# A causal convolution and two gated layers on one core: the convolution's steps spread over both phases of a tile, and eight input buffers allocated at another place

## The chip, the cores and the metric

One core of a Trainium2 chip runs the whole kernel. The metric is the device time of one execution in microseconds (us); less is better. The four compute engines run side by side and are ordered only by semaphores: TensorE (PE, with its weight loads shown apart as PEld), VectorE (DVE), ScalarE (ACT) and GpSimd (POOL). SyncE (SP) issues all DMAs.

## The reference, cut to what matters

```python
# x: 4 x 4096 x 192, weight: 8 x 7 (8 heads of 24 channels, 7 taps)
w = softmax(weight, axis=-1)
x[t, channel] = sum over k of w[head, k] * x[t - 6 + k, channel]   # zero before the sequence
x = x.reshape(16384, 192)
h = x @ w_in1;  x = (h * cos(h)) @ w_out1               # 192 -> 2048 -> 192
h = x @ w_in2;  out = (h * clip(h + 3, 0, 6) / 6) @ w_out2
```

All in float32.

## The kernel before, in words

The 16,384 tokens are cut in 32 tiles of 512. Everything on the chip is transposed: channels (or hidden units) on partitions, 512 tokens along the row. 192 channels are 128 ("main") and 64 ("tail").

**Precision.** Each float32 operand of a product is held as a rounded high part and a low part (the remainder), and a product is made of high x high, low x high and high x low. So `in_f` (float32) gives `in_hi` and `in_lo`, and `in_ftail` gives `in_tail` and `in_twin`; the gated hidden values in `gate` give `g_hi` (by ACT) and `g_lo` (by POOL).

**Phases and slots.** A phase is one layer of one tile, cut in 8 slots (`SLOTS`); a slot makes 2 x 128 of the 2048 hidden units. The order of phases is L1 tile 0, L1 tile 1, L2 tile 0, L1 tile 2, L2 tile 1, and so on: a "turn" k is L1 of tile k followed by L2 of tile k-1 (`turn_phases`). In a slot PE makes the first products (`first_unit`, L374, out to `h_ps`) of this slot and the second products (`main_unit` L381 to `acc`, `tail_unit` L388 to `acc_tail`) of the slot three before (`LAG`). All matmuls use 64 rows of the array, and two of them run at once, one on the lower 64 partitions and one on the upper 64. `phase` on PE walks 19 rounds (`TURNS`) per slot, each round one `lower` and one `upper` matmul; in 18 of the 19, one of the two is a first product and the other a second product. In all there are 512 slots of 19 rounds, 9728 rounds.

**From h to g.** For L1: ACT copies h with a bias to an integer (L523), DVE subtracts (L628), ACT takes the cosine (L533), DVE multiplies (L639). For L2: ACT adds 3 and clips below (L525), DVE clips above and multiplies (L642). Then ACT rounds to `g_hi` (L540) and POOL subtracts to `g_lo` (L794).

**What PE waits for.** Before the first products of a slot PE waits for `g_ready`: DVE must have gated the first half of the slot two before, since `h_ps` has two places. At slot 0 of a phase it also waits for `lo_ready` and `twin_ready`: the phase's inputs must have been split. For L1 of the next tile these are `in_hi`, `in_twin`, `in_tail` (ACT, `split_high`, L552, L555, L558) and `in_lo`, the lower half of `in_tail` (DVE, `split_low_main` L695 and `split_low_tail` L700).

**The convolution.** For each tile DVE transposes the loaded x (`turn_x`, L657 and L658), puts in the 6 columns kept from the tile before (`put_halo`, L672 and L673), and does 14 steps (`conv_taps`): 7 taps, each on main and on tail. Steps 0 and 1 are a product (L683), the other 12 a product and a sum, scalar_tensor_tensor (L687). All of this is placed by hand: in DVE's L2 phase, `turn_x` and `put_halo` behind slot 0's gating, then 3 steps in each of slots 1 to 4 and 2 in slot 5 (`conv_from=1`, `rate=3`). The splits stand at slot 6 (`SPLIT_SLOT = SLOTS - 2`) on ACT and DVE. In slot 3 (`DRAIN_SLOT`) DVE also drains the accumulators of the phase before (`drain_acc`), in slot 7 (`TURN_SLOT`) it transposes a finished output tile (`turn_result`). In the first phase (L1 tile 0) there are 2 steps a slot, with 4 done ahead.

**SP's queue.** In the loop, turn k issues the load of x for tile k+1 and then the store of tile k-2. A load of tile i waits for `x_turned`: x of tile i-1 must have been transposed. A store waits for `o_turned`.

**At the start** the weights are loaded and split, and PE does 10 dummy matmuls (`warm_up`, L499, 128 rows each) between the 9th step of the first convolution and the first product.

**Buffers.** On a partition they lie one behind the other in the order of their allocation, each rounded up to 32 bytes. The weights, `g_hi` and `g_lo` all begin at byte 128 of a 512-byte line. Between them and the split inputs stand `xT` and `xT_tail` (2072 bytes each) and `halo` and `halo_tail` (888 bytes each), so that `in_hi`, `in_lo`, `in_tail` and `in_twin` begin at byte 448. Every slice of weights that PE loads begins a multiple of 512 bytes into its buffer.

Of the kernel before, what the change touches and what calls it, by code (L numbers as in the profile page):

```python
# [14 lines left out]
P = 128  # L15
TOK = 512
LAG = 3
WARM_PRODUCTS = 10
WARM_STEP = 9
# [10 lines left out]
Phase = namedtuple("Phase", "layer tile base before number result convolved conv_from rate setup source")  # L30


def conv_moe_kernel(nc, x, weight, w_in1, w_out1, w_in2, w_out2, out):
# [60 lines left out]
    with ctx:  # L94
# [21 lines left out]
        stage = sb("stage", [P, 2, W])  # L116

# [10 lines left out]
        in_hi = [sb(f"in_hi{n}", [P, TOK], F32R) for n in (1, 2)]  # L128
        in_lo = [sb(f"in_lo{n}", [P, TOK], F32R) for n in (1, 2)]
        in_tail = [sb(f"in_tail{n}", [P, TOK], F32R) for n in (1, 2)]  # L130
        in_twin = [sb(f"in_twin{n}", [P, TOK], F32R) for n in (1, 2)]
# [120 lines left out]
        SPLIT_SLOT = SLOTS - 2  # L252
        TURN_SLOT = SLOTS - 1
        TURNS = 19
        STEPS_AHEAD = 4
# [32 lines left out]

        def first_phase():
            return Phase(L1, 0, 0, None, 0, None, 1, 1, 2, 0, L2)  # L290

        def turn_phases(k):

            base = 2 * SLOTS * k - SLOTS
            first = isinstance(k, int) and k == 1
            last = isinstance(k, int) and k == TILES - 1
            return [Phase(L1, k, base, L1 if first else L2, 2 * k - 1, None, None, None, None,
                          1 if first else None, L1),
                    Phase(L2, k - 1, base + SLOTS, L1, 2 * k, None if first else k - 2,
                          None if last else k + 1, 1, 3, 2 if first else None, L2)]  # L300

        def last_phase():
            return Phase(L2, TILES - 1, END - SLOTS, L2, 2 * TILES - 1, TILES - 2, None, None, None, None, L1)
# [7 lines left out]
        @block.sync  # L311
        def _(sp):
            def load_x(i):

                if not isinstance(i, int) or i > 0:
                    sp.wait_ge(x_turned, 2 * i)
                for b in range(BLOCKS_D):
                    sp.dma_start(chip_block(x_in, x_in_tail, b), dram_block(x_blocks, i, b)).then_inc(x_loaded, 16)

            def load_block(b):  # L320
                for dst, src in loads_of(b):
                    sp.dma_start(dst, src).then_inc(staged[buffer_of(b)], 16)
# [12 lines left out]
            load_x(1)  # L335
            for b in (6, 7):
                sp.wait_ge(wlo_done, b - 5)
                load_block(b)
            for b in (8, 9):
                sp.wait_ge(wlo_done, b - 1)  # L340
                load_block(b)
            load_x(2)
            for b in range(10, 2 * BLOCKS):
                sp.wait_ge(wlo_done, b - 1)
                load_block(b)
            with sp.Fori(2, TILES - 1) as k:
                load_x(k + 1)
                store(k - 2)
            for i in range(TILES - 3, TILES):
                store(i)  # L350
            sp.wait_ge(o_stored, 16 * (BLOCKS_D * TILES + 1))

        @block.tensor
        def _(pe):
# [138 lines left out]

            def warm_up():

                pe.wait_ge(whi_done, 1)
                pe.wait_ge(conv_step, WARM_STEP)
                for _ in range(WARM_PRODUCTS):
                    pe.matmul(h_ps[:, 1, TOK:W], win_hi[L1][:, 0:P], win_hi[L1][:, 0:TOK], start=True, stop=True)  # L499
# [7 lines left out]
            with pe.Fori(2, TILES - 1) as k:  # L507
                for ph in turn_phases(k):
                    phase(ph)
            for ph in turn_phases(TILES - 1):  # L510
                phase(ph)
# [4 lines left out]
        def _(act):  # L516
# [54 lines left out]
            def phase(ph):  # L571
                for q in range(SLOTS):
# [6 lines left out]
                    if ph.convolved is not None and q == SPLIT_SLOT:  # L579
# [33 lines left out]
            with act.Fori(2, TILES - 1) as k:  # L613
                for ph in turn_phases(k):
                    phase(ph)
            for ph in turn_phases(TILES - 1):
                phase(ph)
# [4 lines left out]
        def _(dve):  # L622
# [80 lines left out]
            def phase(ph):  # L703
                for q in range(SLOTS):
# [67 lines left out]
            for n in range(STEPS_AHEAD):  # L772
# [4 lines left out]
            with dve.Fori(2, TILES - 1) as k:  # L777
                for ph in turn_phases(k):
                    phase(ph)
            for ph in turn_phases(TILES - 1):  # L780
                phase(ph)
# [69 lines left out]
```

## Time and profile before

| | us |
|---|---|
| three runs | 2375.68, 2374.58, 2376.42 (median 2375.68) |
| the profiled execution | 2375.52 |
| its span (first to last instruction) | 2373.8 |
| mean granted TensorE clock | 0.997 of full |

| engine | busy us | share of the span | instructions |
|---|---|---|---|
| PE | 2286.3 | 96% | 19470 |
| PEld | 1997.7 | 84% | 19470 |
| DVE | 1851.5 | 78% | 2509 |
| ACT | 1705.8 | 72% | 2836 |
| POOL | 1468.8 | 62% | 1059 |

A matmul's busy time is a modelled 0.39 us, while in a full stream one starts every 0.23 us, so PE shows as busy through short waits; the starts tell more than the shares. A turn of the loop takes 72.36 us.

### The profile page before, as it was taken

Reading aid. Unit: us, or ns where it says so; the run is one execution under the profiler, and the core shown is the slowest. Engines: PE = TensorE matmul, PEld = TensorE weight load, DVE = VectorE, ACT = ScalarE, POOL = GpSimd, SP = SyncE. Lnnn points to the kernel's source line nnn. Section 1 sums busy time; section 2 is a strip of 40 time slices with the busy share of each in tenths; the row PEclk is TensorE's granted clock in tenths of the full one; section 3 lists DMA queues with packets and bytes.
Section 4 is the critical chain, followed back from the end, with each engine's and each line's share of the span. In section 5 each row is a group of like instructions: output and inputs, shape, how many; then the busy total and the mean of one; then the engine's idle time right before and its main releaser. Section 6 shows DMA issues by size and latency. Waiting matters only on the chain.

```text
span 2373.8 us, 57021 instructions
## 1 busy us (share of the span) xinstructions
PE 2286.3 (96%) x19470; PEld 1997.7 (84%) x19470; DVE 1851.5 (78%) x2509; ACT 1705.8 (72%) x2836; POOL 1468.8 (62%) x1059
## 2 busy tenths in 40 slices
PE   5899999999999999999999999999999999999998
PEld 4789798888889888888898888998788988888886
DVE  8688877888877888777888778887778887788853
ACT  5876777766777667777667777677776677776674
POOL 6766666566566666566666665665666666656664
PEclk9999999999999999999999999999999999999999
DMA  4100000000000000000000000000000000000001
GB/s 109 37 8 15 0 13 13 13 13 7 7 13 13 13 13 0 13 13 13 13 9 4 13 13 13 13 0 13 13 13 13 12 1 13 13 13 13 2 7 21
DMA packets 208238, 32.94 MB, mean 14 GB/s; under 512 B 203088, under 2 KB 207184, under 8 KB 208208
## 3 DMA queue, kind: packets, MB, share of 16 engines
q1 hardware_dynamic: 208208, 32.53, 7.8%
q8 instruction: 20, 0.33, 0.1%
q14 instruction: 10, 0.08, 0.0%
HBM read 19.92 MB, written 12.58 MB: 14 GB/s over the span
## 4 chain that ended last, share of the span: by engine, by line
PE 44%; issue 22%; DVE 19%; POOL 9%; ACT 4%; DVEq 1%; POOLq 0%; SPq 0%; DMA 0%; ACTq 0%
PE h_ps L374 18%; PE acc L381 16%; PE acc_tail L388 11%; POOL g_lo L794 9%; DVE in_ftail L687 6%; DVE gate L642 5%; DVE in_f L687 4%; DVE in_f L683 1%; DVE in_tail L700 1%; ACT in_tail L558 1%; DVE in_ftail L651 1%; ACT in_hi L552 1%; ACT in_twin L555 1%; ACT pre L525 1%; ACT g_hi L540 0%
## 5 line engine op out<-in xcount | busy, mean ns | idle before, releaser
L794 POOL TENSOR_TENSOR g_lo<-gate,g_hi 128x512 fp32r<-128x512 f32 x1024 | 1428.9, 1417 | 857.1 <-ACT g_hi L540 855.7
L381 PE MATMUL acc<-g_hi,wout 64*128 64x512 f32 x4096 | 1429.9, 389 | 1.7 <-POOL g_lo L794 1.7
L374 PE MATMUL h_ps<-in_hi,win_hi 64*128 64x512 f32 x2048 | 808.3, 395 | 60.8 <-DVE in_tail L700 46.5
L540 ACT ACTIVATE g_hi<-gate 128x512 fp32r<-128x512 f32 x1024 | 613.7, 631 | 326.4 <-DVE gate L642 275.6
L381 PEld LDWEIGHTS acc<-g_hi,wout 64*128 64x128 f32 x4096 | 756.2, 185 | 66.4 <-issue 3.1
L388 PE MATMUL acc_tail<-g_lo,wout 64*128 64x512 f32 x2048 | 807.4, 394 | 0.0
L388 PE MATMUL acc_tail<-g_hi,wout 64*128 64x512 f32 x2048 | 805.6, 393 | 0.0
L374 PE MATMUL h_ps<-in_lo,win_hi 64*128 64x512 f32 x2048 | 803.2, 392 | 0.0
L374 PE MATMUL h_ps<-in_hi,win_lo 64*128 64x512 f32 x2048 | 800.3, 391 | 0.0
L381 PE MATMUL acc<-g_lo,wout 64*128 64x512 f32 x2048 | 800.2, 391 | 0.0
L374 PE MATMUL h_ps<-in_tail,wtail_hi 64*128 64x512 f32 x2048 | 798.1, 390 | 0.0
L628 DVE TENSOR_TENSOR pre<-pre,h_ps 128x512 f32<-128x512 int32 x512 | 334.6, 684 | 289.5 <-ACT pre L523 288.5
L374 PEld LDWEIGHTS h_ps<-in_hi,win_hi 64*128 64x128 f32 x2048 | 379.1, 185 | 109.8 <-issue 44.7
L525 ACT ACTIVATE pre<-h_ps,three 128x512 f32<-128x512 f32 x512 | 337.2, 683 | 163.8 <-PE h_ps L374 163.1
L642 DVE SCALAR_TENSOR_TENSOR gate<-pre,h_ps 128x512 f32<-128x512 f32 x512 | 332.6, 676 | 126.2 <-ACT pre L525 126.1
L388 PEld LDWEIGHTS acc_tail<-g_lo,wout 64*128 64x128 f32 x2048 | 376.5, 184 | 32.9
L374 PEld LDWEIGHTS h_ps<-in_hi,win_lo 64*128 64x128 f32 x2048 | 378.2, 185 | 27.6
L381 PEld LDWEIGHTS acc<-g_lo,wout 64*128 64x128 f32 x2048 | 376.3, 184 | 29.6
L374 PEld LDWEIGHTS h_ps<-in_lo,win_hi 64*128 64x128 f32 x2048 | 379.2, 185 | 24.8
L388 PEld LDWEIGHTS acc_tail<-g_hi,wout 64*128 64x128 f32 x2048 | 379.3, 185 | 24.5
L374 PEld LDWEIGHTS h_ps<-in_tail,wtail_hi 64*128 64x128 f32 x2048 | 378.6, 185 | 22.4
L533 ACT ACTIVATE pre<-pre,half_pi 128x512 f32<-128x512 f32 x512 | 349.1, 717 | 65.4 <-DVE pre L628 56.2
(72 smaller groups left out, 2359.3 us busy)
## 6 DMA issues: line engine op xcount, KB each, us to landing
x_in<-in_x SPq DMA_DIRECT2D x128, 64.0 KB, 2.2
out_dram<-o_blk SPq DMA_DIRECT2D x128, 64.0 KB, 1.8
blk_tail<-in_x SPq DMA_DIRECT2D x64, 64.0 KB, 2.2
out_dram<-blk_tail SPq DMA_DIRECT2D x64, 64.0 KB, 1.8
stage<-in_moe_w_out SPq DMA_DIRECT2D x6, 384.0 KB, 3.3
stage<-in_moe_w_in SPq DMA_DIRECT2D x3, 512.0 KB, 3.5
stage<-in_moe_w_in SPq DMA_DIRECT2D x6, 256.0 KB, 4.3
gate<-in_moe_w_out SPq DMA_DIRECT2D x2, 384.0 KB, 11.0
```

Of the source, the lines that this page charges most:

```text
L374: return pe.matmul(chunk_of(h_ps, q, half), w, x, start=start, stop=stop)
L381: return pe.matmul(acc[pair][:, :], wout[layer][rows, 2 * q + half, cols], g[rows, :], start=start, stop=stop)
L388: return pe.matmul(acc_tail[pair][:, :], wout[layer][rows, 2 * q + half, P:2 * P], g[rows, :], start=start, stop=stop)
L525: i = act.activation(p, h, ACT.Relu, bias=three[:, 0:1])
L533: act.activation(p, p, ACT.Sin, bias=half_pi[:, 0:1], scale=-TWO_PI).then_inc(cos_ready, 1)
L540: act.activation(chunk_of(g_hi, q, half), chunk_of(gate, q, half), ACT.Copy).then_inc(ghi_ready, 1)
L552: act.activation(in_hi[to][:, :], in_f[layer][:, :], ACT.Copy).then_inc(hi_ready[to], 1)
L555: act.activation(in_twin[to][DT:P, :], in_ftail[layer][:, :], ACT.Copy).then_inc(twin_ready[to], 1)
L628: dve.tensor_tensor(p, p.bitcast(I32), chunk_of(h_ps, q, half), ALU.subtract).then_inc(frac_ready, 1)
L642: dve.scalar_tensor_tensor(out=g, in0=p, scalar=6.0, in1=h, op0=ALU.min, op1=ALU.mult).then_inc(g_ready, 1)
L687: ins = dve.scalar_tensor_tensor(out=dst[:, :], in0=src[:, t:t + TOK], scalar=taps[0:rows, part, t:t + 1], in1=dst[:, :], op0=ALU.mult, op ...
L794: pool.tensor_tensor(chunk_of(g_lo, q, half), chunk_of(gate, q, half), chunk_of(g_hi, q, half).bitcast(F32), ALU.subtract).then_inc(glo_re ...
```

## The change

`conv_from` and `rate` go; a list says how many steps are done before each slot. L1's phases now carry four of the fourteen steps (one each in slots 1, 4, 6 and 7), and L2's phases carry ten (2, 2, 2, 1, 3 in slots 0 to 4). The first phase keeps its steps. The splits stand at slot 5 in place of 6, except in the first phase, where they stay at 6. `turn_x` of tile k+2 stands at the end of turn k (slot 7 of L2, behind `turn_result`), `put_halo` in slot 0 of L1. SP loads x one tile further ahead: tile 3 ahead of the loop, then tile k+2 in turn k, in front of the store. The loops of PE, ACT, DVE and SP end one turn earlier, and that turn is written out. The warm-up starts 2 steps earlier and is 50 pairs of 64-row matmuls, in four series at different places in the buffers, where it was 10 matmuls of 128 rows. The eight split input buffers are allocated in front of `x_in`, and so begin at byte 128 of a 512-byte line.

```diff
-WARM_PRODUCTS = 10
-WARM_STEP = 9
+WARM_STEP = 7
+WARM_SERIES = 10
@@ buffers
         stage = sb("stage", [P, 2, W])
+        in_hi = [sb(f"in_hi{n}", [P, TOK], F32R) for n in (1, 2)]
+        in_lo = [sb(f"in_lo{n}", [P, TOK], F32R) for n in (1, 2)]
+        in_tail = [sb(f"in_tail{n}", [P, TOK], F32R) for n in (1, 2)]
+        in_twin = [sb(f"in_twin{n}", [P, TOK], F32R) for n in (1, 2)]
         x_in = sb("x_in", [P, TOK])
...
         in_ftail = [sb(f"in_ftail{n}", [DT, TOK]) for n in (1, 2)]
-        in_hi = [sb(f"in_hi{n}", [P, TOK], F32R) for n in (1, 2)]
-        in_lo = [sb(f"in_lo{n}", [P, TOK], F32R) for n in (1, 2)]
-        in_tail = [sb(f"in_tail{n}", [P, TOK], F32R) for n in (1, 2)]
-        in_twin = [sb(f"in_twin{n}", [P, TOK], F32R) for n in (1, 2)]
@@ where the steps stand
-        SPLIT_SLOT = SLOTS - 2
+        SPLIT_SLOT = SLOTS - 3
+        CONV_FIRST = [4, 4, 6, 8, 10, 12, 14, 14, 14]
+        CONV = {0: [0, 0, 1, 1, 1, 2, 2, 3, 4], 1: [4, 6, 8, 10, 11, 14, 14, 14, 14]}
+        def conv_range(ph, q):
+            done = CONV_FIRST if ph.setup == 0 else CONV[ph.layer]
+            return range(done[q], done[q + 1])
+        def splits_convolved(ph, q):
+            return ph.convolved is not None and (ph.layer == L2 or ph.setup == 0) and q == split_slot(ph)
+        def split_slot(ph):
+            return SPLIT_SLOT + 1 if ph.setup == 0 else SPLIT_SLOT
@@ SP
-            with sp.Fori(2, TILES - 1) as k:
-                load_x(k + 1)
+            load_x(3)
+            with sp.Fori(2, TILES - 2) as k:
+                load_x(k + 2)
                 store(k - 2)
@@ PE
+            def warm_units(moving_at, weights_at):
+                for rows, dst in ((LOW, acc[1][:, :]), (UP, h_ps[:, 1, TOK:W])):
+                    pe.matmul(dst, win_hi[L1][rows, weights_at:weights_at + P],
+                              win_hi[L1][rows, moving_at:moving_at + TOK], start=True, stop=True)
             def warm_up():
-                pe.wait_ge(whi_done, 1)
+                pe.wait_ge(whi_done, 2)
                 pe.wait_ge(conv_step, WARM_STEP)
-                for _ in range(WARM_PRODUCTS):
-                    pe.matmul(h_ps[:, 1, TOK:W], win_hi[L1][:, 0:P], win_hi[L1][:, 0:TOK], start=True, stop=True)
+                for _ in range(2 * WARM_SERIES):
+                    warm_units(0, HALF_FF - 2 * P)
+                for _ in range(WARM_SERIES):
+                    warm_units(16, HALF_FF - 2 * P)
+                for _ in range(WARM_SERIES):
+                    warm_units(0, HALF_FF - 2 * P + 16)
+                for _ in range(WARM_SERIES):
+                    warm_units(16, HALF_FF - 2 * P + 16)
@@ DVE, in a slot of a phase
-                        if ph.setup != 0 and q == 0:
-                            turn_x(ph.convolved)
+                        if ph.layer == L1 and ph.setup != 0 and q == 0:
                             put_halo(ph.convolved)
-                        n = (q - ph.conv_from) * ph.rate + (STEPS_AHEAD if ph.setup == 0 else 0)
-                        if q >= ph.conv_from:
-                            for m in range(n, min(n + ph.rate, len(STEPS))):
-                                conv_taps(ph.convolved, m)
-                        if q == SPLIT_SLOT:
+                        for m in conv_range(ph, q):
+                            conv_taps(ph.convolved, m)
+                        if splits_convolved(ph, q):
...
                     if ph.result is not None and q == TURN_SLOT:
                         turn_result(ph.result, result_turn(ph))
+                    if ph.turned is not None and q == TURN_SLOT:
+                        turn_x(ph.turned)
```

## Rows read from the trace of the kernel before

**Rows 1.** The waits of all engines: who waited for whom, total us, times, longest.

```profile
PE h_ps L374 <- DVE in_tail L700: 46.5, 33, 7.1
...
PEld h_ps L374 <- DVE gate L642: 26.7, 30, 0.9
```

**Rows 2.** PE's timeline over one turn: start us, duration us, what ran [idle before].

```profile
1019.21 0.48 PE L374 MATMUL h_ps<-in_hi,win_hi 64*128 64x512 f32 x1 [1.11 <-DVE in_tail L700]
...
1084.94 0.39 PE L388 MATMUL acc_tail<-g_hi,wout 64*128 64x512 f32 x1
...
1085.83 0.49 PE L374 MATMUL h_ps<-in_hi,win_hi 64*128 64x512 f32 x1 [0.45 <-DVE gate L642]
...
1086.17 0.38 PE L374 MATMUL h_ps<-in_lo,win_hi 64*128 64x512 f32 x1
...
1090.07 0.39 PE L388 MATMUL acc_tail<-g_hi,wout 64*128 64x512 f32 x1
...
1091.59 0.49 PE L374 MATMUL h_ps<-in_hi,win_hi 64*128 64x512 f32 x1 [1.13 <-DVE in_tail L700]
```

**Rows 3.** DVE's timeline in an L2 phase of tile 12, slots 0 to 6.

```profile
986.21 0.69 DVE L642 SCALAR_TENSOR_TENSOR gate<-pre,h_ps 128x512 f32<-128x512 f32 x1 [1.27 <-ACT pre L525]
...
987.76 0.70 DVE L657 STREAM_TRANSPOSE xT<-x_in 128x512 f32<-128x512 f32 x1
...
996.91 0.74 DVE L687 SCALAR_TENSOR_TENSOR in_ftail<-xT_tail,taps,in_ftail 64x512 f32<-64x512 f32 x1
997.58 1.78 DVE L687 SCALAR_TENSOR_TENSOR in_f<-xT,taps,in_f 128x512 f32<-128x512 f32 x1
...
1012.72 1.27 DVE L642 SCALAR_TENSOR_TENSOR gate<-pre,h_ps 128x512 f32<-128x512 f32 x2
...
1018.37 0.69 DVE L700 TENSOR_TENSOR in_tail<-in_ftail,in_tail 64x512 fp32r<-64x512 f32 x1 [0.21 <-ACT in_tail L558]
```

**Rows 4.** PE's timeline in the last turn and behind it.

```profile
2249.43 0.50 PE L374 MATMUL h_ps<-in_hi,win_hi 64*128 64x512 f32 x1 [1.02 <-DVE in_tail L700]
...
2354.97 0.39 PE L388 MATMUL acc_tail<-g_lo,wout 64*128 64x512 f32 x1
...
2356.12 0.39 PE L381 MATMUL acc<-g_hi,wout 64*128 64x512 f32 x1
```

**Rows 5.** DVE's, POOL's and PE's timelines in an L1 phase.

```profile
1043.64 1.30 DVE L639 TENSOR_TENSOR gate<-pre,h_ps 128x512 f32<-128x512 f32 x2 [0.20 <-ACT pre L533]
1046.65 1.28 DVE L628 TENSOR_TENSOR pre<-pre,h_ps 128x512 f32<-128x512 int32 x2 [1.70 <-ACT pre L523]
...
1045.13 2.56 POOL L794 TENSOR_TENSOR g_lo<-gate,g_hi 128x512 fp32r<-128x512 f32 x2 [2.26 <-ACT g_hi L540]
...
1045.68 0.39 PE L374 MATMUL h_ps<-in_hi,win_hi 64*128 64x512 f32 x1
```

**Rows 6.** DVE's and PE's timelines at the start.

```profile
13.77 0.73 DVE L687 SCALAR_TENSOR_TENSOR in_f<-xT,taps,in_f 128x512 f32<-128x512 f32 x1
...
29.66 0.79 PE L374 MATMUL h_ps<-in_hi,win_hi 64*128 64x512 f32 x1 [7.07 <-DVE in_tail L700]
...
42.21 0.39 PE L374 MATMUL h_ps<-in_tail,wtail_hi 64*128 64x512 f32 x1
...
42.90 0.39 PE L374 MATMUL h_ps<-in_hi,win_lo 64*128 64x512 f32 x1
```

**Rows 7.** PE's timeline at two early waits, and busy times with the granted clock (PEclk).

```profile
72.54 0.79 PE L374 MATMUL h_ps<-in_hi,win_hi 64*128 64x512 f32 x1 [3.15 <-DVE in_tail L700]
...
76.97 0.62 PE L388 MATMUL acc_tail<-g_lo,wout 64*128 64x512 f32 x1
...
77.39 0.62 PE L388 MATMUL acc_tail<-g_hi,wout 64*128 64x512 f32 x1
...
113.56 0.50 PE L374 MATMUL h_ps<-in_hi,win_hi 64*128 64x512 f32 x1 [2.96 <-DVE in_tail L700]
...
75.00:78.00 3.00, 3.00 (x18) 2.35 (x16) 0.36 (x1) 1.97 (x3) 0.96 (x1) 0.50 0.00 0
```

More of the change, by code:

```diff
@@ L22 @@
 HALF_PI = float(np.float32(np.pi / 2))
-Phase = namedtuple("Phase", "layer tile base before number result convolved conv_from rate setup source")
+Phase = namedtuple("Phase", "layer tile base before number result turned convolved setup source")
 def conv_moe_kernel(nc, x, weight, w_in1, w_out1, w_in2, w_out2, out):
@@ L251, in conv_moe_kernel @@
         DRAIN_SLOT = LAG
-        SPLIT_SLOT = SLOTS - 2
+        SPLIT_SLOT = SLOTS - 3
         TURN_SLOT = SLOTS - 1
+        CONV_FIRST = [4, 4, 6, 8, 10, 12, 14, 14, 14]
+        CONV = {0: [0, 0, 1, 1, 1, 2, 2, 3, 4], 1: [4, 6, 8, 10, 11, 14, 14, 14, 14]}
         TURNS = 19
-        STEPS_AHEAD = 4
         L1, L2 = 0, 1
@@ L287, in splits_of @@
             return ph.tile + 1 + (ph.source == L2)
+        def conv_range(ph, q):
[5 more added lines that the diff above has]
+            return SPLIT_SLOT + 1 if ph.setup == 0 else SPLIT_SLOT
         def first_phase():
-            return Phase(L1, 0, 0, None, 0, None, 1, 1, 2, 0, L2)
+            return Phase(L1, 0, 0, None, 0, None, 2, 1, 0, L2)
         def turn_phases(k):
@@ L296, in turn_phases @@
             last = isinstance(k, int) and k == TILES - 1
[L297 to L300, printed above, removed]
+            more = None if last else k + 1
+            late = isinstance(k, int) and k + 2 >= TILES
+            return [Phase(L1, k, base, L1 if first else L2, 2 * k - 1, None, None, more, 1 if first else None, L1),
+                    Phase(L2, k - 1, base + SLOTS, L1, 2 * k, None if first else k - 2, None if late else k + 2,
+                          more, 2 if first else None, L2)]
         def last_phase():
-            return Phase(L2, TILES - 1, END - SLOTS, L2, 2 * TILES - 1, TILES - 2, None, None, None, None, L1)
+            return Phase(L2, TILES - 1, END - SLOTS, L2, 2 * TILES - 1, TILES - 2, None, None, None, L1)
         def splits_last(ph, q):
@@ L345, in _ @@
                 load_block(b)
-            with sp.Fori(2, TILES - 1) as k:
-                load_x(k + 1)
+            load_x(3)
+            with sp.Fori(2, TILES - 2) as k:
+                load_x(k + 2)
                 store(k - 2)
-            for i in range(TILES - 3, TILES):
+            for i in range(TILES - 4, TILES):
                 store(i)
@@ L506, in _ @@
                 phase(ph)
-            with pe.Fori(2, TILES - 1) as k:
+            with pe.Fori(2, TILES - 2) as k:
                 for ph in turn_phases(k):
                     phase(ph)
-            for ph in turn_phases(TILES - 1):
-                phase(ph)
+            for k in (TILES - 2, TILES - 1):
+                for ph in turn_phases(k):
+                    phase(ph)
             phase(last_phase())
@@ L578, in phase @@
                         cosine(q, SLOTS * ph.tile + q)
-                    if ph.convolved is not None and q == SPLIT_SLOT:
+                    if splits_convolved(ph, q):
                         act.wait_ge(conv_step, len(STEPS) * (ph.convolved + 1))
@@ L612, in _ @@
                 phase(ph)
-            with act.Fori(2, TILES - 1) as k:
+            with act.Fori(2, TILES - 2) as k:
                 for ph in turn_phases(k):
                     phase(ph)
-            for ph in turn_phases(TILES - 1):
-                phase(ph)
+            for k in (TILES - 2, TILES - 1):
+                for ph in turn_phases(k):
+                    phase(ph)
             phase(last_phase())
@@ L714, in phase @@
                     if ph.convolved is not None:
-                        if ph.setup != 0 and q == 0:
-                            turn_x(ph.convolved)
+                        if ph.layer == L1 and ph.setup != 0 and q == 0:
                             put_halo(ph.convolved)
-                        n = (q - ph.conv_from) * ph.rate + (STEPS_AHEAD if ph.setup == 0 else 0)
-                        if q >= ph.conv_from:
-                            for m in range(n, min(n + ph.rate, len(STEPS))):
-                                conv_taps(ph.convolved, m)
-                        if q == SPLIT_SLOT:
+                        for m in conv_range(ph, q):
+                            conv_taps(ph.convolved, m)
+                        if splits_convolved(ph, q):
                             split_low_main(L1, L1, ph.convolved - 1)
@@ L771, in _ @@
             put_halo(1)
-            for n in range(STEPS_AHEAD):
+            for n in range(CONV_FIRST[0]):
                 conv_taps(1, n)
@@ L776, in _ @@
                 phase(ph)
-            with dve.Fori(2, TILES - 1) as k:
+            with dve.Fori(2, TILES - 2) as k:
                 for ph in turn_phases(k):
                     phase(ph)
-            for ph in turn_phases(TILES - 1):
-                phase(ph)
+            for k in (TILES - 2, TILES - 1):
+                for ph in turn_phases(k):
+                    phase(ph)
             phase(last_phase())
```

## The prediction

> **What bounds the kernel now.** I read the page's busy shares first: PE is at 96%, but a matmul is shown as 0.39 us long while the next starts sooner, so the share hides short waits. The waits of all engines show two kinds at PE that come back every turn: 33 for `in_tail` of DVE L700, 46.5 us in all, and 30 for `gate` of DVE L642, 26.7 us [rows 1]. PE's timeline gives their true size by the starts of rounds. In a turn one wait stands from 1084.94 to 1085.83 and one from 1090.07 to 1091.59; the round behind each takes 0.34 (1085.83 to 1086.17) [rows 2]. From 1019.21 to 1091.59 is one turn, 72.38 us; over 17 turns, from 1019.21 to 2249.43, it is 72.366 [rows 2, 4].
>
> A turn without them can be read off too. Behind 2249.43 no tile is left to be convolved, and PE has no wait until 2354.97, which is 24 slots later: (105.54 - 0.10 for the slow first round) / 24 = 4.393 us a slot, 0.2312 a round [rows 4]. Sixteen slots are 70.29. So PE sets the pace in all but 72.37 - 70.29 = 2.08 us of each turn, and there DVE does, in L2's slots alone.
>
> Why DVE is late: the first scalar_tensor_tensor behind a gating takes 0.74, the next 1.78 [rows 3], because it starts while POOL makes `g_lo`. Following starts overlap by 0.07 (997.58 - 996.91 = 0.67 for the 0.74), so a slot with three steps costs DVE 1.2 (gating) + 0.67 + 1.70 + 1.70 = 5.3 us of a slot of 4.39. Slot 0's gating starts at 986.21; undelayed, slot 5's would at 986.21 + 5 x 4.393 = 1008.2, but starts at 1012.72, and PE, which wants its first half two slots later, stands until then. The same queue brings the last split only at 1018.37 + 0.69 = 1019.06, and PE starts at 1019.21 [rows 2, 3].
>
> (The Trainium skill, SBUF — State Buffer, "SBUF: two separate sides", says that a DVE instruction with two SBUF inputs and a GpSimd one that reads SBUF share a port pair which the first to start holds for its whole length. The trace agrees, 0.74 against 1.78. By it the moved steps are cheap only where DVE starts before POOL, which is the condition of rival B below.)
>
> **The change, part by part.**
>
> *Steps out of L2.* DVE per slot becomes 1.2 + 0.67 + 1.70 = 3.6 us in slots 0 to 2, about 3.3 in slot 3 (one step and the drain, two instructions of some 0.7), 5.3 in slot 4, and some 2.6 in slot 5 (gating, two splits). Only slot 4 is over 4.39, by 0.9. How much lateness does PE stand? The gating at 1085.08 (1012.72 plus a turn) would have had to give its first half before 1085.17, where PE's round was due; it takes 0.65, so it had to start by 1084.5, which in the shown turn is 1012.1: 3.9 us behind the undelayed 1008.2 [rows 2, 3]. 0.9 of 3.9 is used: the wait for `gate` goes. The steps end at about 986.21 + 4 x 4.393 + 5.3 = 1009.1; ACT's three splits and DVE's last low one, at 0.69 each, end at about 1011.9, where PE would want them at 1017.0 (1019.21 less the 2.08 of both waits, less 0.1 for the slow round). The second wait goes, with 5 us to spare. ACT's `g_hi` of slot 5 comes 2 us later, behind which wait POOL's `g_lo` and, three slots on, the second products: no price.
>
> *Steps into L1.* There, ACT and DVE answer each other, and between a slot's last gating and the next subtraction DVE is idle for 1.70 [rows 5]. A step put there starts at 1044.9, before POOL's `g_lo` at 1045.13, so it should cost 0.67 (steps 0 and 1, with one SBUF input, 0.5) and POOL is put back by up to 0.5, out of 2.26 idle. Even a blocked one, 1.78, is over by 1046.7 against 1046.65. Slots 1, 4, 6, 7 carry one each. L1 stands less lateness than L2: the first half of slot 4's gating ends at 1043.64 + 0.65 = 1044.3, PE uses it at 1045.68: 1.4 us [rows 5]. `put_halo` in slot 0 takes 0.5 to 1.3, also in an idle stretch. Price 0; bounds 0 and 0.7 us a turn (a whole blocked step beyond its gap, less the slack left).
>
> *turn_x at the end of the turn.* Two transposes, 0.7 each [rows 3], behind `turn_result`. Undelayed, slot 7's gating ends at 1018.6, the four transposes at 1021.4. L1's first subtraction is due at about 1017.0 + 13 rounds (3.0) + a matmul (0.4) + ACT's copy (some 0.6) = 1021.0: 0.4 late inside a slack of 1.4. Price 0. The load it waits for was issued a turn earlier; SP's queue passes `store` only once, and nothing on the chip waits for the load for 70 us. The written-out turn adds instructions, no work.
>
> *So per turn* -2.08. The wait for `gate` comes 30 times and, the one at 113.56 and its like at the start aside, so does that for `in_tail`: 30 x 2.08 = -62.4.
>
> *The start.* The seventh step ends at 14.5, so 50 warm pairs start there. At the slow clock a round takes 0.43 (76.97 to 77.39, granted clock 0.50), in a full stream 0.23 [rows 2, 7]. Behind 72.54 the slow clock lasted beyond 77.39, where a matmul still took 0.62: some 5.3 us of paired matmuls. So about 12 slow pairs and 38 fast ones: 5.3 + 8.8 = 14.1, over at 28.6, ahead of the first products at 29.66 [rows 6]. Bounds: all slow, 21.5 us, ends at 36.0, +6.3. If it ends in time, the first products find the full clock, where before they had 0.79 at 29.66 and 0.39 only by 42.21 [rows 6]; but the first subtraction has DVE's own steps before it, so only the second half's chain gains, some 1 to 2 us. I take -1.5. Later, `in_tail` of L2 tile 0 (PE waited 2.96 us until 113.56 [rows 7]) is put back by the step now standing before it in slot 6, 0.7 to 1.7: +1. Both early waits may again be followed by a slow clock or not: between -2.5 and +2.5.
>
> *The place of the buffers.* No row shows first products at byte 128. What stands near: second products, which have it already (`g_hi`, `g_lo`, `wout`), run alone behind 2354.97 and need (2356.12 - 2354.97) / 5 = 0.230 a round [rows 4]; first products alone at byte 448 need (42.90 - 42.21) / 3 = 0.230 [rows 6]. Each round but one in 19 holds one of either kind, and starts both together at 0.2312. A misplaced operand that cost something would show in the second row. I take 0. Bounds: between the two waits of a turn 17 rounds took 3.90 us, 0.2294 each [rows 2], which over 9728 rounds is -18; as much the other way, +18. The far ends, half of a slow round (0.2135) and the 0.34 behind a wait, make rivals C and D.
>
> Sum against the profiled execution: 2375.5 - 62.4 - 1.5 + 1.0 = 2312.6. It lies 0.2 under the median of the runs, so 2312.7 there.
>
> **Rivals.**
>
> *A, forecast, 0.74:* 2312.7, its own range 2306 to 2322.
>
> *B, a wait comes back in L1, 0.12.* If POOL starts before DVE's moved step in most slots, the lateness adds up to more than 1.4 us and PE stands 0.7 us a turn: +21, 2334. For it: L1's slack is a third of L2's. Against it: DVE's gating ends 0.2 us before POOL starts, and the gaps are 1.2 to 1.7 us.
>
> *C, the place frees the round, 0.07.* Half of a slow round (77.39 - 76.97 = 0.42 to 0.43 [rows 7]) says 0.2135 for a bare one; the 0.0177 above that is unexplained. Were all of it due to the first products' place, 9728 x 0.0177 = -172, 2141; a fifth of it gives 2278. Against: the second products alone are no faster. (The Trainium skill, TensorE: Matmul & The Clock Gate, "Wait — 56ns, not 53.3ns?", gives 215.7 ns start to start for 512 columns at the full clock. No run here shows it; by it the sum would be 2162.)
>
> *D, the other side, 0.04: the place costs.* Both operands of both halves then ask the same part of a line at the same time, in every round. It decides at 63 / 9728 = 6.5 ns a round, 0.2377; a tenth of the way to 0.34, 0.242, gives 2418. Against: the second products need 0.230 at that very place.
>
> *E, 0.03: the waits stay* since something behind DVE sets them: 2374. Against: both end within 0.2 us of DVE's instruction.
>
> **How the numbers follow.** Predicted is A's time. The range 2285 to 2336 leaves out most of C below, and E, D and the far end of B above, about 0.15. This kernel's runs tell 0.2% (5 us) from no change. Slower is D, 0.04; same is E, 0.03; faster is the rest, 0.93.
>
> **What would show it.** Right: no wait of PE on `in_tail` or `gate` behind 120 us; a turn of 70.3 us; PE's idle time (span less busy), now 87.5, under 45; in L1, moved steps of 0.74 with POOL starting just behind them; the warm pairs over by 29.6 and first products from there on at 0.23. Wrong: the turn over 70.5 without a wait means that the round has changed, and the mean start to start in a turn tells by how much; a wait of PE in L1's slots is B; moved steps of 1.78 say that POOL starts first; first products later than 29.7 say that the warm-up is too long.

## The result: 2281.05 us, faster than forecast

| | us |
|---|---|
| before, median of 4 runs | 2375.85 |
| changed kernel, median of 4 runs (2279.71 to 2281.67) | 2281.05 |
| ratio | 0.9601, 95% interval 0.9584 to 0.9618 |
| forecast | 2312.7, range 2285 to 2336 |

The direction was right. The size was not: the time lies 31.7 us below the forecast and 4 us below the range. One of the four runs of a later experiment, the one with the old warm-up, took 2500.44 us at a granted clock of 0.85 and is left out of its time. Lines of the page of the changed kernel follow; PE's lines of code stand 16 further down in it than before, those of the other engines 29 or 30.

```profile
span 2279.3 us, 56966 instructions
...
PE 2245.0 (98%) x19560; PEld 1842.9 (81%) x19560; DVE 1811.7 (79%) x2509; ACT 1722.4 (76%) x2836; POOL 1509.4 (66%) x1059
```

PE's idle time is 2279.3 - 2245.0 = 34.3 us, under the 45 that I had named. The waits of PE and of its weight loads (us in total, times, longest) answer to [rows 1]:

```profile
PEld h_ps L390 <- DVE gate L669: 17.6, 62, 0.8
...
PE h_ps L390 <- DVE in_tail L730: 10.7, 3, 4.7
...
PE h_ps L390 <- DVE gate L669: 0.8, 2, 0.5
```

The 33 waits for `in_tail` are 3, all at the start, and the 30 for L2's `gate` (L642 before, L672 now) are gone. So far it went as forecast. New are 62 short waits of the weight loads for L1's `gate` (L669); what they cost is told below, at put_halo. The turn was not as forecast: PE's timeline, same place in two turns, answers to [rows 2]:

```profile
1149.27 0.39 PE L397 MATMUL acc<-g_hi,wout 64*128 64x512 f32 x1
...
1149.54 0.50 PE L390 MATMUL h_ps<-in_hi,win_hi 64*128 64x512 f32 x1
...
1149.88 0.39 PE L390 MATMUL h_ps<-in_lo,win_hi 64*128 64x512 f32 x1
...
1218.71 0.50 PE L390 MATMUL h_ps<-in_hi,win_hi 64*128 64x512 f32 x1
```

A turn is 1218.71 - 1149.54 = 69.17 us, where 72.37 was and 70.29 was forecast. The two waits of before held only 2.08, so the other 1.1 us are no wait that went: it is the round itself, the case that I had named for a turn off its value without waits. The number of matmuls in a fixed stretch of the loop says by how much (columns: stretch, us, then busy us and instructions of PE, PEld, DVE, ACT, POOL, then granted clock, DMA share, GB/s). The changed kernel:

```profile
217.00:2110.00 1893.00, 1893.00 (x16644) 1554.62 (x16642) 1541.37 (x2136) 1457.81 (x2408) 1262.20 (x876) 1.00 0.07 11
```

Two matmuls make a round: 1893 / (16644 / 2) = 0.2275 us, with all that is left of waits in it; between the waits it is 0.2268. The granted clock is 1.00 in this stretch. So the question was what made a round 3.7 ns shorter than 0.2312. I took it to the chip with the place of the buffers as the suspect (theory "place") and the moved DVE steps as the rival (theory "no waits": PE is no longer stopped twice a turn, and its stream is smoother for it).

### The profile page after: what moved, and what is told of

Same layout as the page of the kernel before. It is cut to its first block, busy times and chain, and to the rows that moved or that the text cites. A ratio compares the mean times of both kernels' runs of the same rounds, so it can differ in the third digit from the quotient of the medians.

```text
span 2279.3 us, 56966 instructions
## 1 busy us (share of the span) xinstructions
PE 2245.0 (98%) x19560; PEld 1842.9 (81%) x19560; DVE 1811.7 (79%) x2509; ACT 1722.4 (76%) x2836; POOL 1509.4 (66%) x1059
## 4 chain that ended last, share of the span: by engine, by line
PE 94%; DVE 3%; ACT 2%; issue 0%; SPq 0%; DMA 0%; DVEq 0%; ACTq 0%
PE h_ps L390 45%; PE acc L397 30%; PE acc_tail L404 20%; ACT pre L562 1%; DVE gate L669 1%; DVE pre L658 1%; ACT g_hi L569 1%; DVE in_ftail L717 1%; DVE in_f L717 1%; ACT pre L552 0%; DVE in_tail L730 0%; DMA blk_tail<-in_x 0%; SPq L333 0%; ACT wout L598 0%; ACT in_hi L581 0%
## 5 line engine op out<-in xcount | busy, mean ns | idle before, releaser
L824 POOL TENSOR_TENSOR g_lo<-gate,g_hi 128x512 fp32r<-128x512 f32 x1024 | 1469.0, 1456 | 722.2 <-ACT g_hi L569 721.8
L390 PE MATMUL h_ps<-in_hi,win_hi 64*128 64x512 f32 x2048 | 798.7, 391 | 11.8 <-DVE in_tail L730 10.7
L404 PE MATMUL acc_tail<-g_lo,wout 64*128 64x512 f32 x2048 | 797.6, 389 | 0.0
L390 PE MATMUL h_ps<-in_lo,win_hi 64*128 64x512 f32 x2048 | 792.9, 387 | 0.0
L404 PE MATMUL acc_tail<-g_hi,wout 64*128 64x512 f32 x2048 | 792.4, 387 | 0.0
L397 PE MATMUL acc<-g_lo,wout 64*128 64x512 f32 x2048 | 791.7, 387 | 0.0
L554 ACT ACTIVATE pre<-h_ps,three 128x512 f32<-128x512 f32 x512 | 344.9, 685 | 224.5 <-PE h_ps L390 224.5
L672 DVE SCALAR_TENSOR_TENSOR gate<-pre,h_ps 128x512 f32<-128x512 f32 x512 | 339.1, 681 | 188.0 <-ACT pre L554 178.7
```

What stands on the lines that cost most here:

```text
L390: return pe.matmul(chunk_of(h_ps, q, half), w, x, start=start, stop=stop)
L397: return pe.matmul(acc[pair][:, :], wout[layer][rows, 2 * q + half, cols], g[rows, :], start=start, stop=stop)
L404: return pe.matmul(acc_tail[pair][:, :], wout[layer][rows, 2 * q + half, P:2 * P], g[rows, :], start=start, stop=stop)
L554: i = act.activation(p, h, ACT.Relu, bias=three[:, 0:1])
L672: dve.scalar_tensor_tensor(out=g, in0=p, scalar=6.0, in1=h, op0=ALU.min, op1=ALU.mult).then_inc(g_ready, 1)
L824: pool.tensor_tensor(chunk_of(g_lo, q, half), chunk_of(gate, q, half), chunk_of(g_hi, q, half).bitcast(F32), ALU.subtract).then_inc(glo_re ...
```

## Experiments

Each ratio is to the kernel before, run on the same chip, with its 95% interval.

**The place taken back.** The changed kernel, with the eight split inputs where they were.

```diff
-        in_hi = ...; in_lo = ...; in_tail = ...; in_twin = ...     # behind stage
         in_ftail = [sb(f"in_ftail{n}", [DT, TOK]) for n in (1, 2)]
+        in_hi = ...; in_lo = ...; in_tail = ...; in_twin = ...     # byte 448 again
```

> The changed kernel with the eight split input buffers back behind in_ftail, at byte 448 of a 512-byte line; all else stays. Theory 'place': the round goes back from 0.2275 us to about 0.2312, so 9728 x 0.0037 = +36 us, 2317, and the two PE streams start 13 to 36 ns apart again. Theory 'no waits' (the round fell because PE is no longer stopped twice a turn): the round stays at 0.2275 and the time at 2281.

Measured: 2315.77 us (2315.58 to 2316.24), 0.9751 [0.9735, 0.9768]. The same stretch of the loop, and two starts a turn apart from PE's timeline:

```profile
217.00:2110.00 1893.00, 1893.00 (x16378) 1654.31 (x16376) 1522.51 (x2101) 1429.26 (x2370) 1218.22 (x864) 1.00 0.07 11
```

```profile
1100.16 0.39 PE L390 MATMUL h_ps<-in_hi,win_hi 64*128 64x512 f32 x1
...
1170.45 0.39 PE L390 MATMUL h_ps<-in_hi,win_hi 64*128 64x512 f32 x1
```

The turn is 70.29 us and the round 1893 / 8189 = 0.2312, both as forecast. So my sum was right for this kernel (2312.7 against 2315.8), and the place alone is worth 2315.77 - 2281.05 = 34.7 us, 3.6 ns on each of 9728 rounds. Nothing is left for the rival: the schedule is the same in both kernels.

**The place alone.** The kernel before, with only the inputs moved.

> The kernel before with only the eight split input buffers moved to byte 128 of a line. Theory 'place': the round falls to about 0.2268 in the stretches without a wait; but DVE's late slots in L2 stay as long as they were, so PE waits longer there and only L1's half and the last turns keep the gain: 2375.9 less 15 to 36, about 2350. Theory 'no waits': 2376, round 0.2312.

Measured: 2335.46 us (2332.7 to 2336.41), 0.983 [0.9814, 0.9846], some 15 us under what I expected. PE's waits in it, and the one for `gate` in the kernel before:

```profile
PE h_ps L374 <- DVE in_tail L700: 48.9, 33, 8.3
...
PE h_ps L374 <- DVE gate L642: 14.7, 31, 1.2
```

```profile
PE h_ps L374 <- DVE gate L642: 13.6, 30, 0.5
```

The steady waits stay, the round between them falls to 0.2269, and 40 us go. I had thought that a shorter round would be paid back in longer waits, since DVE sets the L2 phase. They hardly grew, because DVE's own share of the phase fell too: from the gating of slot 0 to that of slot 5 it took 26.5 us before and takes 25.3 here. Most of this is one instruction, the first product of the convolution. It takes 1.54 before and 0.47 here, in every turn of the loop:

```profile
992.15 1.54 DVE L683 TENSOR_SCALAR in_f<-xT,taps 128x512 f32<-128x512 f32 x1
```

```profile
1119.31 0.47 DVE L683 TENSOR_SCALAR in_f<-xT,taps 128x512 f32<-128x512 f32 x1
```

That was not planned, so part of the 40 us is luck of the phase. Place and schedule each help without the other: 40 and 59 us alone, 95 together, nearly their sum.

**Which places count.** Behind the warm-up 23 series of 40 rounds are put in, on `win_hi`'s own data. The weights begin at element 1024 of it, the moving operand at element d; the product goes to PSUM places that are overwritten later. Everything else is as in the changed kernel.

```diff
+    for d in (0, 1, 2, 4, 8, 16, 24, 32, 48, 64, 80, 96, 112, 124, 127, 128, 256):
+        series([(LOW, low, d, 1024), (UP, up, d, 1024)])       # both halves of the rows
+    ...                                                        # one half moved; one stream; 128 rows
```

> The changed kernel with 23 series of 40 rounds of dummy products behind the warm-up, weights at a fixed place and the moving operand d elements (4 bytes each) further: d = 0, 1, 2, 4, 8, 16, 24, 32, 48, 64, 80, 96, 112, 124, 127, 128, 256 for both streams, then lower 0 with upper 0 or 80, then one stream alone and then 128 rows at once, each with 0 and 80. Only the time between starts in the trace counts, not the run's time. Theory 'place': 0.2267 at d = 0, 128 and 256 (same place in 512 bytes), 0.229 to 0.236 at the others, also for one stream alone. Theory 'no waits': 0.2267 throughout, since nothing is waited for in any series.

Mean start to start in the second half of each series (ns), by d in elements of 4 bytes (the series ran once; 1024 elements are a multiple of 512 bytes):

| d | 0 | 1 | 2 | 4 | 8 | 16 | 24 | 32 | 48 |
|---|---|---|---|---|---|---|---|---|---|
| ns | 226.6 | 236.6 | 233.5 | 231.8 | 233.4 | 229.1 | 233.2 | 233.2 | 233.5 |

| d | 64 | 80 | 96 | 112 | 124 | 127 | 128 | 256 |
|---|---|---|---|---|---|---|---|---|
| ns | 226.6 | 228.9 | 232.0 | 233.4 | 236.5 | 226.7 | 226.6 | 226.7 |

Three of these can be read off PE's timeline. First d = 0 and d = 1, ten rounds each, (42.02 - 39.75) / 10 = 0.227 and (52.05 - 49.69) / 10 = 0.236:

```profile
39.75 0.39 PE L533 MATMUL acc<-win_hi 64*128 64x512 f32 x1
...
42.02 0.39 PE L533 MATMUL acc<-win_hi 64*128 64x512 f32 x1
...
49.69 0.40 PE L533 MATMUL acc<-win_hi 64*128 64x512 f32 x1
...
52.05 0.40 PE L533 MATMUL acc<-win_hi 64*128 64x512 f32 x1
```

Then d = 64, which is 256 bytes, again ten rounds, 0.226:

```profile
124.75 0.39 PE L533 MATMUL acc<-win_hi 64*128 64x512 f32 x1
...
127.01 0.39 PE L533 MATMUL acc<-win_hi 64*128 64x512 f32 x1
```

With d = 0 for one half of the rows and 80 for the other, the first needs 226.6 and the other 228.95: each stream pays for its own. One stream alone needs 226.7 (d = 0) and 228.9 (d = 80). On all 128 rows it is the same, here as merged rows of 12 matmuls: (2.88 - 0.39) / 11 = 0.2264 and (2.91 - 0.39) / 11 = 0.2291.

```profile
233.78 2.88 PE L533 MATMUL h_ps<-win_hi 128*128 128x512 f32 x12
...
243.81 2.91 PE L533 MATMUL h_ps<-win_hi 128*128 128x512 f32 x12
```

So it is not a conflict between the two halves: what counts is how far the moving operand stands from the weights, and it repeats every 256 bytes (within 0.2 ns at 0, 64 and 192 bytes, within 1.2 at 128). I had expected 512 and a slow round at d = 64. The weights stayed at one place in these series; the warm-up of the changed kernel, read in the next section, moves them too.

**Two shifts in the real kernel.** A pad of 64 bytes, and one of 256, ahead of the inputs.

```diff
+        pad = sb("pad", [P, 16])      # in the other kernel [P, 64]
         in_hi = ...
```

> The changed kernel with an unused buffer of 64 bytes in front of the split inputs, which so begin at byte 192 against 128 for the weights. Theory 'place': the round goes back to 0.231 to 0.233, 2310 to 2330. Theory 'no waits': 2281. A third theory, that only 320 bytes apart is bad, or the distance to other buffers matters: also 2281.

Measured: 2316.11 us (2312.81 to 2316.76), 0.9748 [0.9731, 0.9764]. Its round, 1893 / (16378 / 2), is 0.2312:

```profile
217.00:2110.00 1893.00, 1893.00 (x16378) 1858.49 (x16376) 1522.54 (x2101) 1429.02 (x2371) 1218.16 (x864) 1.00 0.07 11
```

> The changed kernel with an unused buffer of 256 bytes in front of the split inputs (byte 384 of a 512-byte line, weights at 128). The series of dummy products had 0.2266 at 0, 256, 512 and 1024 bytes and 0.229 to 0.237 in between. If the place within 256 bytes decides: 2281, round 0.2275. If the place within 512 bytes does after all, in the real stream of changing weights: 2316, as with 64 or 320 bytes.

Measured: 2279.86 us (2278.65 to 2280.79), 0.9601 [0.9585, 0.9617]. The same stretch of the loop gives a round of 1893 / (16642 / 2) = 0.2275, as in the changed kernel, and a turn is 69.18:

```profile
217.00:2110.00 1893.00, 1893.00 (x16642) 1554.35 (x16640) 1542.76 (x2138) 1457.44 (x2409) 1261.89 (x875) 1.00 0.07 11
```

64 bytes lose the whole gain, 256 lose nothing: the change puts the inputs at the weights' place in a 512-byte line, but the same place in 256 bytes is enough. In the bare series 64 bytes cost 2.5 ns, in the kernel some 4.4 (0.2312 against 0.2268). The series have no second kind of product in between; whether that makes the difference was not tried.

**The steps back into L2.** The transposes of x and the splits stay as in the change, but no step goes to L1.

```diff
-        CONV = {0: [0, 0, 1, 1, 1, 2, 2, 3, 4], 1: [4, 6, 8, 10, 11, 14, 14, 14, 14]}
+        CONV = {0: [0] * 9, 1: [0, 3, 6, 9, 11, 14, 14, 14, 14]}
```

> The changed kernel with all 14 steps in L2's slots 0 to 4 (3, 3, 3, 2, 3), none in L1; early turn_x and splits at slot 5 stay. If L2's lateness is what the spreading cured: slots 0 to 2 and 4 cost DVE 5.3 us of 4.31, slot 3 some 5.0, so DVE is about 4.7 late at slot 5, over the 3.7 to 3.9 that PE stands: a wait for gate of 0.8 to 1 us a turn, in_tail not waited for, 2281 + 25 to 30 = 2306 to 2311; put_halo still in L1. If the early transposes and the split at slot 5 alone were enough: 2281 or, as L1 loses its steps, 2275.

Measured: 2272.04 us (2269.2 to 2272.7), 0.9563 [0.9547, 0.9579]. The turn is 68.92, and the steady waits have not come back. DVE in slot 0 of L2:

```profile
1155.08 0.55 DVE L713 TENSOR_SCALAR in_f<-xT,taps 128x512 f32<-128x512 f32 x1
1155.54 1.51 DVE L713 TENSOR_SCALAR in_ftail<-xT_tail,taps 64x512 f32<-64x512 f32 x1
1156.98 0.73 DVE L717 SCALAR_TENSOR_TENSOR in_f<-xT,taps,in_f 128x512 f32<-128x512 f32 x1
1157.64 0.67 DVE L672 SCALAR_TENSOR_TENSOR gate<-pre,h_ps 128x512 f32<-128x512 f32 x1
```

These three take 1157.64 - 1155.08 = 2.56 us, not the 0.67 + 1.70 + 1.70 = 4.07 that I had charged three steps: only one of the three is long. Slots 1, 2 and 4 do take the 5.3 with their gating. From the gating of slot 0 to that of slot 5 DVE needs 24.3 us here against 26.5 before. That makes it 24.3 - 5 x 4.31 = 2.8 late at slot 5, which is under the 3.7 to 3.9 that PE can bear. So L2 is cured by what this experiment keeps: the two transposes and put_halo out of slot 0, steps in slot 0 in their place, two steps and not three beside the drain in slot 3, and the splits in slot 5. Which of these is enough alone was not tried. The part of the change that moves four steps into L1 was not needed, and this version is 9 us below the changed kernel; the next experiment says where they come from.

**put_halo out of L1.** In the changed kernel DVE's timeline shows, in slot 0 of L1 and in slot 1 behind it:

```profile
1126.34 1.28 DVE L703 COPY halo<-xT 128x6 f32 x1
1127.53 0.15 DVE L702 COPY xT_tail<-halo_tail 64x6 f32 x1
1127.61 1.26 DVE L703 COPY halo_tail<-xT_tail 64x6 f32 x1
1128.78 1.27 DVE L658 TENSOR_TENSOR pre<-pre,h_ps 128x512 f32<-128x512 int32 x2
...
1131.47 0.48 DVE L713 TENSOR_SCALAR in_f<-xT,taps 128x512 f32<-128x512 f32 x1
```

```profile
1126.28 2.56 POOL L824 TENSOR_TENSOR g_lo<-gate,g_hi 128x512 fp32r<-128x512 f32 x2 [3.21 <-ACT g_hi L569]
```

Copies of 6 columns take 0.15 us, or 1.28 beside POOL's `g_lo`: 2.6 in all where I had put 0.5 to 1.3, and the subtraction starts behind them. The moved step costs 0.48 as forecast. In this experiment the transposes of x stand in L2's slot 5, behind the splits, and put_halo in slot 6.

```diff
-    if ph.layer == L1 and ph.setup != 0 and q == 0:
+    if ph.setup == 1 and q == 0:
         put_halo(ph.convolved)
...
-    if ph.turned is not None and q == TURN_SLOT:
+    if ph.turned is not None and q == (TURN_SLOT if ph.setup == 0 else SPLIT_SLOT):
         turn_x(ph.turned)
+    if ph.turned is not None and ph.setup != 0 and q == SPLIT_SLOT + 1:
+        put_halo(ph.turned)
```

> The changed kernel with turn_x of the next tile in slot 5 of L2 (behind the splits) and put_halo in slot 6, in place of slot 7 and L1's slot 0. In the changed kernel put_halo took 2.6 us in L1 (1126.27 to 1128.87, two of its four copies 1.27 each beside POOL's g_lo), ACT waited 1.03 us behind it, and PE waits for gate in L1's slots 6 and 7, 0.26 us a turn. If put_halo is the cause: these waits go, a turn of 68.91, 30 x 0.26 = -8, 2273. If ACT's own load in L1 (4.0 us a slot and four extra instructions of 0.6) is enough to make PE wait at this faster round: 2279 to 2281.

Measured: 2273.1 us (2272.7 to 2273.93), 0.9572 [0.9556, 0.9588]. The turn is 68.91 us, sixteen slots of 19 rounds of 0.2267, with no round over 0.25 in the loop. The four copies take 0.36 together. This experiment moved the transposes too, but the one with the steps back in L2 helps to part the two. There put_halo still stands in L1's slot 0, and it happens to run ahead of POOL, in every turn:

```profile
1122.07 0.17 DVE L702 COPY xT<-halo 128x6 f32 x1
...
1122.29 0.15 DVE L703 COPY halo_tail<-xT_tail 64x6 f32 x1
```

The copies are short in both, and the turn is 68.9 in both. With the steps left in L1 and put_halo out of it (this experiment) 8 of the 9 us come back, so the moved steps by themselves cost 1 us or nothing. The last 0.26 us of the changed kernel's turn was rival B in small: put_halo beside POOL made L1 late, and PE stood for 0.05 to 0.11 at three rounds a turn (one is 1149.54 to 1149.88 above). It did so only at the faster round. With the place taken back the copies take the same 2.6, and at 0.2312 no round of the loop is over 0.25.

**The start: the warm-up.** The changed kernel with the 10 dummy matmuls of before, behind the 9th step.

> The changed kernel with the warm-up of before (10 products of 128 rows, behind the 9th step). If the longer warm-up is worth what the first slots of the two traces show (slow rounds until 37 against 40.3, the wait at 57 to 59 about 1.2 us earlier): 2281 + 1 to 2. If it is worth nothing, since DVE and ACT set the first phase: 2281.

Measured: 2280.94 us (2280.18 to 2282.1 in three runs), 0.9605 [0.9585, 0.9624]. The new warm-up is worth nothing that these runs can tell.

**The start: three more kernels.** The first has put_halo in L2, 62 warm pairs at one place, and a list of its own for the second phase.

```diff
+        CONV_SECOND = [0, 0, 2, 3, 3, 4, 4, 4, 4]
-    for _ in range(2 * WARM_SERIES): ...      # and the three other series
+    for _ in range(WARM_PAIRS):               # 62
+        warm_units(0, HALF_FF - 2 * P)
```

> As the one before, and at the start: 62 warm pairs at one place in place of 50 (the 50 ended at 26.8 and the first products at 29.68 found the slow clock), and in the second phase the four convolution steps in slots 1, 2 and 4 (2, 1, 1), none in slot 6 ahead of the low split that PE waits for. If both costs are as read: the first products at the full clock, some 1 us; the wait at 108.7 shorter by the 1.8 of the step ahead of the split, and with less than 4 us perhaps no slow clock behind it (2.4 us): 2273 less 3 to 5, about 2269. If the start is bound by DVE and ACT alone: 2273.

Measured: 2270.64 us (2270.2 to 2271.9), 0.9563 [0.9547, 0.9579], 2.5 us below the kernel with put_halo in L2 alone. Which of the two new parts gives them was not tried. The changed kernel's wait of 4.67 us (its row stands in the section on the start below) is 1.66 shorter, and still there:

```profile
111.88 0.49 PE L391 MATMUL h_ps<-in_hi,win_hi 64*128 64x512 f32 x1 [3.01 <-DVE in_tail L725]
```

The second adds to it `CONV_FIRST = [4, 6, 8, 10, 12, 14, 14, 14, 14]` and splits a slot earlier in the first phase.

> The kernel with put_halo in L2 and the mended start (e8_halo_start), and in the first phase the convolution steps one slot earlier (two in each of slots 0 to 4) and the splits at slot 5 in place of 6. PE waits 3.65 us at 67.1 for in_tail there, with slow rounds behind it until about 74. If DVE can do the steps earlier in its idle time of slot 0: the wait goes and so do the slow rounds, 3 to 5 us, 2266. If DVE has no room (its odd slots are full with POOL splitting weights): PE waits as long for gate in earlier slots, 2270.

Measured: 2270.0 us (2268.92 to 2271.34), 0.9559 [0.9543, 0.9574]. The wait near 68 went from 3.65 to 1.95 us start to start, but it ends at 71.45 where it ended at 70.74, because the slots before it took longer (a wait of 1.5 us in front of 38.8 is new): no gain that can be told. The third also has the splits of the second phase a slot earlier.

```diff
-        SPLIT_AFTER_DRAIN = {"hi": 4, "twin": 4, "tail": 5, "low_main": 5, "low_tail": 6}
+        SPLIT_AFTER_DRAIN = {"hi": 4, "twin": 4, "tail": 4, "low_main": 5, "low_tail": 5}
```

> As e10_first_split, and in the second phase ACT makes in_tail in slot 4 in place of 5 and DVE its low half in slot 5 in place of 6. PE waits 3.4 us at 108.5 for it. If that order is the cause: 3 us and perhaps the slow clock behind it less, 2 to 5 under e10. If ACT's load of the second phase is (weights, three splits, 4.1 us of every slot): the wait moves to gate in slots 5 to 7 and the time stays.

Measured: 2268.22 us (2265.24 to 2268.39), 0.9548 [0.9532, 0.9564]. It is the best of all, 12.8 us under the changed kernel, and the intervals of the two do not meet. Most of that, 8 us, is put_halo out of L1. The start gives the other 5; the runs with and without it lie apart (2265.24 to 2268.39 against 2272.7 to 2273.93), but their ratio intervals overlap, as do those of the three start kernels with each other.

## Why the prediction was wrong

**The step that failed: "The place of the buffers … I take 0."** It measures -34.7 us. The sum without it gave 2312.7, and the kernel without it runs in 2315.8. The direction is that of rival C, to which I gave 0.07; its sum for a fifth of the unexplained 17.7 ns, 2278, is close to what came, but the fifth was picked and not worked out, so that this is luck. The bound of -18 us was too narrow as well.

The argument failed in its reading of two rows. I held that second products, which already had the good place, run alone at 0.230 [rows 4], no faster than first products at the old place [rows 6]. In the changed kernel the very same second products, at the very same place, in the same stretch behind the last turn:

```profile
2260.53 0.39 PE L404 MATMUL acc_tail<-g_lo,wout 64*128 64x512 f32 x1
...
2261.67 0.39 PE L397 MATMUL acc<-g_hi,wout 64*128 64x512 f32 x1
```

Five rounds in 1.14 us, 0.228 each, against 1.15, 0.230, in [rows 4]. The traces hold nanoseconds, and there the same five rounds take 0.2268 each in the changed kernel and 0.2310 before. So four rows at a resolution of 0.01 us were read as saying that a place does nothing. They stood for three and five rounds, and in the traces read here a stream needs about as many rounds behind a wait or a change of place before it is steady (the last section has the numbers). Those second products came straight out of a stream mixed with badly placed ones. That this is why they were slow is likely but not shown. The 17 rounds at 0.2294 between the two waits, which I used only as a bound, stay unexplained: over the loop the kernel before needs 0.2310 between its waits.

The warm-up of the changed kernel, which I had before me as code but no row of, would have told, and it shows that the absolute place does not count: it runs the four combinations one behind the other. Weights and moving at one place, nine rounds from 17.61 to 19.65 (0.2267); moving operand 64 bytes on, ten rounds from 19.88 to 22.18 (0.230); weights 64 bytes on instead, which puts the moving operand at -64 bytes, ten to 24.52 (0.234; the series had 233.5 and 233.4 ns at d = 48 and 112, the same distance modulo 256); both 64 bytes on, six from 25.22 to 26.58 (0.2267).

```profile
17.61 0.39 PE L513 MATMUL h_ps<-win_hi 64*128 64x512 f32 x1
...
19.65 0.39 PE L513 MATMUL h_ps<-win_hi 64*128 64x512 f32 x1
...
19.88 0.39 PE L513 MATMUL h_ps<-win_hi 64*128 64x512 f32 x1
...
22.18 0.39 PE L513 MATMUL h_ps<-win_hi 64*128 64x512 f32 x1
...
24.52 0.39 PE L513 MATMUL h_ps<-win_hi 64*128 64x512 f32 x1
...
25.22 0.39 PE L513 MATMUL h_ps<-win_hi 64*128 64x512 f32 x1
...
26.58 0.39 PE L513 MATMUL h_ps<-win_hi 64*128 64x512 f32 x1
```

(The Trainium skill, TensorE: Matmul & The Clock Gate, "Wait — 56ns, not 53.3ns?", gives 215.7 ns start to start. No trace here shows it: the shortest steady round in any of them is 226.6, the 2162 that went by it lay 119 us below the measured time, and the gap stays unexplained.)

**The waits: right.** -2.08 us a turn was forecast; the place taken back has 72.37 - 70.29 = 2.08. But the credit was given to the wrong part. I counted steps taken out of L2, and the experiment that leaves all 14 there has no steady wait either. My account of why DVE was late charged every slot with three steps 5.3 us and left out two things: slot 0, where the transposes and put_halo made 4.2 us with the gating, and slot 3, where three steps and the drain made 6.5. (In the paragraph on turn_x slot 7's gating would end at 986.21 + 7 x 4.393 + 1.2 = 1018.2 by the shown rows, and not at 1018.6; nothing rests on it.)

**The moved steps: right.** In L1 a step is 0.48 (above) or 0.74, and POOL starts behind it, as I had said it must:

```profile
1153.98 0.74 DVE L717 SCALAR_TENSOR_TENSOR in_f<-xT,taps,in_f 128x512 f32<-128x512 f32 x1
```

```profile
1154.25 2.89 POOL L824 TENSOR_TENSOR g_lo<-gate,g_hi 128x512 fp32r<-128x512 f32 x2 [1.01 <-ACT g_hi L569]
```

**put_halo: too small.** 0.5 to 1.3 forecast, 2.6 measured, since two of its copies met POOL; worth 0.26 us a turn, some 8 us in all, which the experiment with it in L2 gave back.

**turn_x at the end: right.** The two transposes start at 1122.05 and 1122.68 and the next subtraction at 1123.27, with no wait of PE.

**The start: wrong in what its parts are worth.** The warm pairs are over at 27.0, in time. PE then stands, and the first products run mostly one at a time. In the profiled execution the granted clock falls to 0.59 in the stretch from 29.6 to 38.0:

```profile
29.76 0.49 PE L390 MATMUL h_ps<-in_hi,win_hi 64*128 64x512 f32 x1 [2.79 <-DVE in_tail L730]
```

```profile
29.60:38.00 8.40, 8.24 (x32) 6.56 (x32) 7.72 (x14) 2.58 (x6) 3.86 (x4) 0.59 0.62 146
...
113.80:119.00 5.20, 5.20 (x24) 4.09 (x26) 3.15 (x5) 3.25 (x5) 1.99 (x2) 0.50 0.00 0
```

The fast clock alone would not have helped. With the same warm-up the granted clock is 1.00 in that stretch in the trace of the kernel with put_halo in L2, and there PE is sooner through its first products and then stands for DVE's gating:

```profile
38.17 0.49 PE L390 MATMUL h_ps<-in_hi,win_hi 64*128 64x512 f32 x1 [1.66 <-DVE gate L669]
```

By 43.0 PE has started as many matmuls in the one kernel as in the other. So DVE sets the first phase, and -1.5 became nothing. The later wait, 2.96 before [rows 7], became longer, since the step in front of the split took 1.81 and the split itself 1.63 behind POOL:

```profile
110.20 1.81 DVE L717 SCALAR_TENSOR_TENSOR in_f<-xT,taps,in_f 128x512 f32<-128x512 f32 x1
112.04 1.63 DVE L730 TENSOR_TENSOR in_tail<-in_ftail,in_tail 64x512 fp32r<-64x512 f32 x1
```

```profile
113.73 0.79 PE L390 MATMUL h_ps<-in_hi,win_hi 64*128 64x512 f32 x1 [4.67 <-DVE in_tail L730]
```

That is 4.67 - 2.96 = 1.7 us more, but PE came to the wait 1.5 us earlier, and this gain is gone in it: the wait ends at 113.73, where it ended at 113.56. New is what stands behind it, some 12 rounds at the granted clock of 0.50 (the second of the window rows), each some 0.2 longer: 2.4. Before, the clock was 1.00 there. So the two terms together, -1.5 and +1.0, became 0.2 + 2.4 = +2.6, 3.1 more than forecast. The old place has the same wait (it ends at 113.72) and the same slow rounds behind it; for it the sum would have been 2312.7 + 3.1 = 2315.8, and 2315.77 was measured.

## What to carry to other kernels

Let the moving operand and the weights of a matmul begin at the same place modulo 256 bytes. With 512 columns of float32 nearly all the other places tried cost 1 to 4% of a matmul at the full clock here, and one line of the allocation decides it. Where a kernel is bound by thousands of equal rounds, measure the round over hundreds of them: 3.6 ns is below what three or five rows can show and was 35 us. When a wait goes, undo the parts one at a time before crediting one. Here the steps in L1 were not needed, and the copies that came to stand beside POOL cost 8 us.

## What the hardware showed that I had not expected

- The round depends on the distance of moving operand and weights modulo 256 bytes: 226.6 to 226.7 ns at 0 and at -4 bytes, 229 at +64, 231.8 to 233.5 at most others, 236.6 at +4 and 236.5 at -16. It holds for one stream, for two and for 128 rows. What in the chip makes it was not found.
- At the granted clock of 0.50 a pair takes 0.427 with the inputs at the old place as at the new; the cost shows at the full clock alone.
- Behind a wait or a change of place some three to five rounds, most of them of 0.228 to 0.236, pass before the stream is back at 0.2267. Behind the wait that ends at 113.73, once the clock is back, they are 235, 224, 231, 236 and 228 ns.
- A copy of 6 columns on DVE takes 0.15 us, or 1.28 where it meets POOL's `g_lo`: eight times, where a 512-column step is 2.4 times as long (0.74 and 1.78). A product with one SBUF input takes 0.47 to 0.55 or 1.51 to 1.54.
